# First heads of a hashed attention kernel: loads and row copies moved between queues and engines, clearings moved back, idle products on TensorE

## The chip, the cores and the metric
The kernel runs on one core of a Trainium2 chip. The metric is the device time of one execution in microseconds (us), the median of several runs. TensorE (PE) does the products, VectorE (DVE), ScalarE (ACT) and GpSimd (POOL) the elementwise work, and SyncE (SP) issues nearly all DMAs.

## The reference
```
q_bits, k_bits = (q @ proj > 0), (k @ proj > 0)        # 6 bits, a bucket number for each row
scores = where(q_bucket == k_bucket, q @ k.T / 8, -1e9)
attn = exp(scores - rowmax);  attn /= sum(attn) + 1e-9
x = attn @ v                                           # 2 batches x 8 heads, 768 rows, 64 columns
x = elu(x @ w_in) @ w_out                              # 1536 tokens, 512 -> 2048 -> 512
x = x + routed expert (top 1 of 8, 512 -> 1024 -> 512), for tokens with x @ w_skip > 0
```
All data are f32. Products that need more than one pass's precision are made of a rounded high part and a low part (the rest), both of type fp32r.

## The kernel before, in words
The 16 heads are worked one after the other, in a software pipeline in which the score products of head h stand beside the maxima of head h+1 and the transposes of head h+2. Each engine has an instruction list written out by hand; semaphores order them.

For one head the steps are these. SP loads q and k side by side into `qk_nat` (line 317, `load_qk`). PE transposes them into PSUM, six 128x128 transposes (unit T, line 1160). ACT rounds the transposed pair into `hi` (`round_qk`, line 656), and DVE subtracts it from the PSUM values into `lo` (`low_qk`, line 825). PE multiplies by the projection split into `pw[0]` and `pw[1]` (unit BITS, lines 1167 to 1169, six products of 384 columns), and DVE turns the signs into rows of +-numbers in `qb` and `kb` (`bits`, line 837, two instructions). Meanwhile six row copies move halves of `hi` and `lo` to other partitions, as DMAs on SP's queue: `copy_rows` (line 337) makes `qb`, `kb`, `qa`, `ka` from `hi`, and `copy_low_rows` (line 343) fills the other half of `qa` and `ka` from `lo`. PE then forms six tiles of hashed scores (units MAX, line 1176, two products each) from which DVE takes row maxima (`maximum`, line 845). DVE pads them (`row_maxima`, line 852), PE transposes them (MAX_T, line 1181) and DVE writes them negated into rows of `qb` (`minus_maxima`, line 858). Only then come the true score products (lines 1191, 1192), ACT's exponentials (line 673), and the products with v (lines 1207 to 1209).

All units T, BITS, MAX, MAX_T and SCORES share three pairs of PSUM banks in the order of `PSUM_ORDER`: a unit waits until the third unit before it has been consumed. Round `round_qk(h)` and `low_qk(h)` overwrite `hi` and `lo`, so both wait until all six row copies of head h-1 have landed (`rows_copied`, 16 for each DMA) and until BITS of h-1 is done.

Ahead of the steady pipeline stands a start: FIRST_UNITS on PE (T of head 0, BITS of head 0, T of head 1, six MAX of head 0, MAX_T, BITS of head 1), with DVE in the order `low_qk(0)`, `bits(0)`, `low_qk(1)`, six maxima. Before that, POOL makes the identity and constants (lines 461 to 480, `const_ready`), clears parts of `qb`, `kb` of heads 1 and 2 (line 486) and sets rows of ones (line 490), then clears or sets parts of `p_lo`, `v_hi`, `v_lo` (lines 493 to 497). DVE clears `pw` and the parts of head 0 (lines 800 to 804), and splits the projection into high and low parts, four times a pair of small instructions (lines 811 and 813). SP issues the loads in the order q0, k0, proj twice, q1, k1, v0, v1.

The functions in the program:

Of the kernel before, what the change touches and what calls it, by code (L numbers as in the profile page):

```python
# [5 lines left out]
F32 = mybir.dt.float32  # L6
# [5 lines left out]
ALU = mybir.AluOpType  # L12
ACT = mybir.ActivationFunctionType
AX = mybir.AxisListType

P = 128
# [3 lines left out]
QT = S // P  # L20
HALF = S // 2
BITS = 6
# [37 lines left out]
def head_units(h, s):  # L60
# [8 lines left out]

FIRST_UNITS = [("T", 0, 0), ("BITS", 0, 0), ("T", 1, 0)] + [("MAX", 0, t) for t in range(QT)] + \  # L70
              [("MAX_T", 0, 0), ("BITS", 1, 0)]


PSUM_ORDER = list(FIRST_UNITS)
# [6 lines left out]
def build(nc, q, k, v, proj, w_in, w_out, w_skip, w_gate, w1, w2, out, y_rows):  # L81
    ctx = ExitStack()
    with ctx:
# [132 lines left out]

        names = []

        names += "const_loaded gates_loaded const_step const_ready rows_ready proj_step proj_ready table_in consts2 row_step".split()

        names += "tq_done hi_done lo_done pj_done bits_done m_done max_done mx_ready mt_done neg_done".split()

        names += "v_high v_ready st_done exp_done p_hi_ready p_lo_dve p_lo_pool pv_done eps_ready od_ready".split()

# [29 lines left out]
        def pool_settled(eng):  # L254


            if eng is nc.gpsimd:
                eng.sem_inc(s_["pool_passed"], 1)

        def psum(kind, h, i):  # L260

# [50 lines left out]
        def _(sp):  # L312
            def load_qk(h):
                if h >= 2:
                    sp.wait_ge(s_["tq_done"], h - 1)
                for i, x in enumerate((q_h, k_h)):
                    sp.dma_start(qk_nat[h % 2][:, :, i, :], x[h]).then_inc(qk_loaded[h % 2], 16)

            def load_v(h):
# [10 lines left out]
            def copy_rows(h):  # L330
                i = h % 3
                if h >= 3:
                    sp.wait_ge(s_["st_done"], QT * (h - 2))
                sp.wait_ge(s_["hi_done"], h + 1)
                for dst, src in ((qb[i][0:D, :], hi[0:D, :]), (kb[i][0:D, :], hi[D:P, :]),
                                 (qa[i][D:P, :], hi[0:D, :]), (ka[i][0:D, :], hi[D:P, :])):
                    sp.dma_start(dst.bitcast(F32), src.bitcast(F32)).then_inc(rows_copied[i], 16)

            def copy_low_rows(h):
                i = h % 3  # L340
                sp.wait_ge(s_["lo_done"], h + 1)
                for dst, src in ((qa[i][0:D, :], lo[0:D, :]), (ka[i][D:P, :], lo[D:P, :])):
                    sp.dma_start(dst.bitcast(F32), src.bitcast(F32)).then_inc(rows_copied[i], 16)

            def load_den(pair):
# [18 lines left out]
                    .then_inc(s_["rden_loaded"], 16)  # L364

            load_qk(0)
            for half in range(2):
                sp.dma_start(pj[half * D:half * D + D, :], proj).then_inc(s_["const_loaded"], 16)
            load_qk(1)
            load_v(0)  # L370
            load_v(1)
# [88 lines left out]
        def _(pool):  # L460
# [20 lines left out]
                               fill=TINY, base=BITS - 1, pattern=[[0, 1]], channel_multiplier=-1)\  # L481
                .then_inc(s_["const_ready"], 1)
            pool.wait_ge(s_["const_ready"], 1)
            for i in (1, 2):
                for x in (qb[i], kb[i]):
                    done = pool.memset(x[D:P, :].bitcast(F32), 0.0)
                done.then_inc(s_["const_step"], 1)
                pool.wait_ge(s_["const_step"], 4 + i)
            for i in (1, 2):
                done = pool.memset(kb[i][NEG_ROW:NEG_ROW + QT, :].bitcast(F32), 1.0)  # L490
            done.then_inc(s_["rows_ready"], 1)
            pool.wait_ge(s_["rows_ready"], 2)
            pool.memset(p_lo[:, :, :, HALF:WIDE].bitcast(F32), 0.0)
            for u in range(2):
                at = D * (1 - u)
                pool.memset(v_hi[u][:, :, at:at + D].bitcast(F32), 1.0)
                done = pool.memset(v_lo[u][:, :, at:at + D].bitcast(F32), 0.0)
            done.then_inc(s_["const_step"], 1)
            pool.wait_ge(s_["const_step"], 7)

            def low_of_v(h):

# [146 lines left out]
        def _(act):  # L649
            def round_qk(h):  # L650

                act.wait_ge(s_["tq_done"], h + 1)
                if h:
                    act.wait_ge(rows_copied[(h - 1) % 3], 96 * ((h - 1) // 3 + 1))
                    act.wait_ge(s_["pj_done"], h)
                act.activation(hi[:, :].rearrange("p (b n) -> p b n", b=2), psum("T", h, 0), ACT.Copy)\
                    .then_inc(s_["hi_done"], 1)
# [26 lines left out]
            def outputs(h):  # L684
# [5 lines left out]
                if h >= 4:  # L690
                    act.wait_ge(s_["xt_ready"], (h - 4) // 2 + 1)
                act.activation(o_den[h % 4][:, :].rearrange("p (b n) -> p b n", b=2), ps_o, ACT.Identity,  # L692
                               bias=eps_sum[:, h % 2:h % 2 + 1]).then_inc(s_["od_ready"], 1)

            act.wait_ge(s_["const_ready"], 1)
            act.activation(table[:, :], thr[:, :], ACT.Copy).then_inc(s_["table_in"], 1)
            round_qk(0)
            round_qk(1)
            act.wait_ge(s_["const_step"], 7)
            high_of_v(0)  # L700
            high_of_v(1)

# [94 lines left out]
        def _(dve):  # L797
# [4 lines left out]
                dve.memset(x[D:P, :].bitcast(F32), 0.0).then_inc(s_["proj_step"], 1)  # L802
            dve.wait_ge(s_["proj_step"], 4)
            dve.memset(kb[0][NEG_ROW:NEG_ROW + QT, :].bitcast(F32), 1.0).then_inc(s_["rows_ready"], 1)
            dve.wait_ge(s_["const_loaded"], 32)

            for i, signs in enumerate(((1.0, -1.0), (-1.0, 1.0))):
                rows = slice(i * D, i * D + D)
                for n, sign in enumerate(signs):
                    at = slice(i * K_BITS + n * BITS, i * K_BITS + n * BITS + BITS)  # L810
                    dve.tensor_scalar(pw[0][rows, at], pj[rows, :], sign, None, ALU.mult).then_inc(s_["proj_step"], 1)
                    dve.wait_ge(s_["proj_step"], 4 + 2 * i + n + 1)
                    done = dve.scalar_tensor_tensor(pw[1][rows, at], pj[rows, :], sign, pw[0][rows, at].bitcast(F32),
                                                    ALU.mult, ALU.subtract)
            done.then_inc(s_["proj_ready"], 1)
# [3 lines left out]
            def low_qk(h):  # L819

                dve.wait_ge(s_["hi_done"], h + 1)
                if h:
                    dve.wait_ge(rows_copied[(h - 1) % 3], 96 * ((h - 1) // 3 + 1))
                    dve.wait_ge(s_["pj_done"], h)
                dve.tensor_tensor(lo[:, :].rearrange("p (b n) -> p b n", b=2), psum("T", h, 0),
                                  hi[:, :].rearrange("p (b n) -> p b n", b=2).bitcast(F32), ALU.subtract)\
                    .then_inc(s_["lo_done"], 1)

            def bits(h):

                i = h % 3
                dve.wait_ge(s_["pj_done"], h + 1)
                if h >= 3:
                    dve.wait_ge(s_["st_done"], QT * (h - 2))
                for dst, row in ((qb[i], 0), (kb[i], K_BITS)):
                    rows = slice(row, row + 2 * BITS)
                    done = dve.tensor_scalar(dst[BIT_ROW:BIT_ROW + 2 * BITS, :].rearrange("p (b n) -> p b n", b=2),  # L837
                                             psum("BITS", h, 0)[rows], thr[rows, 0:1], thr[rows, 1:2],
                                             ALU.is_ge, ALU.mult)
                done.then_inc(s_["bits_done"], 1)  # L840
# [37 lines left out]

            low_qk(0)
            bits(0)  # L880
            low_qk(1)
            for t in range(QT):
                maximum(0, t)
            row_maxima(0)
            minus_maxima(0)
            bits(1)
# [259 lines left out]
        def _(pe):  # L1146
# [7 lines left out]
            def prepare(kind, h, i):  # L1154
# [8 lines left out]
                elif kind == "BITS":  # L1163
                    pe.wait_ge(s_["lo_done"], h + 1)
                    for b in range(2):
                        half = slice(b * HALF, b * HALF + HALF)
                        pe.matmul(to[:, b, :], pw[0][:, :], hi[:, half], start=True, stop=False)
                        pe.matmul(to[:, b, :], pw[0][:, :], lo[:, half], start=False, stop=False)
                        mm = pe.matmul(to[:, b, :], pw[1][:, :], hi[:, half], start=False, stop=True)
                    mm.then_inc(s_["pj_done"], 1)  # L1170
                elif kind == "MAX":
                    if i == 0:
                        pe.wait_ge(s_["bits_done"], h + 1)
                        pe.wait_ge(rows_copied[h % 3], 96 * (h // 3 + 1))
                    for b in range(2):
                        mm = pe.matmul(to[:, b, :], qb[h % 3][0:NEG_ROW, i * P:i * P + P],  # L1176
                                       kb[h % 3][0:NEG_ROW, b * HALF:b * HALF + HALF], start=True, stop=True)
                    mm.then_inc(s_["m_done"], 1)
                else:
                    pe.wait_ge(s_["mx_ready"], h + 1)  # L1180
                    pe.transpose(to[:, 0, 0:P], mxp[:, :], ident[:, :]).then_inc(s_["mt_done"], 1)

            def scores(h, s):
# [2 lines left out]
                to = take("SCORES", h, s)  # L1186
                if s == 0:
                    pe.wait_ge(s_["neg_done"], h + 1)
                for b in range(2):
                    half = slice(b * HALF, b * HALF + HALF)  # L1190
                    pe.matmul(to[:, b, :], ka[i][:, s * P:s * P + P], qa[i][:, half], start=True, stop=False)  # L1191
# [20 lines left out]

            pe.wait_ge(s_["const_ready"], 1)
            for unit in FIRST_UNITS:
                if unit[0] == "BITS":
                    pe.wait_ge(s_["proj_ready"], 1)
                elif unit == ("MAX", 0, 0):
                    pe.wait_ge(s_["rows_ready"], 2)
                prepare(*unit)

            for n in range(QT * HEADS):
# [211 lines left out]
```

## Time and profile before

| | us |
|---|---|
| median of three runs | 685.39 |
| lowest and highest | 683.17, 687.35 |
| the profiled execution's own time | 682.89 |
| its span, first to last instruction | 681.1 |

The profile's page gives the busy time of each engine over the span, and then the span in 40 slices of 17 us each. It says that PE is busy for 643.4 us (94%), DVE for 53%, ACT for 48% and POOL for 37%. The first slice is the one that differs: PE is at 3 tenths there. The granted clock of TensorE is written in tenths of full speed. The chain of waits follows the work that ended last back to the start, and names for each stretch the engine and line that the end depended on. One line of a view can stand for several instructions (xN).

### The profile page before, as it was taken

Reading aid. Unit: us, or ns where it says so; the run is one execution under the profiler, and the core shown is the slowest. Engines: PE = TensorE matmul, PEld = TensorE weight load, DVE = VectorE, ACT = ScalarE, POOL = GpSimd, SP = SyncE. Lnnn points to the kernel's source line nnn. Section 1 sums busy time; section 2 is a strip of 40 time slices with the busy share of each in tenths; the row PEclk is TensorE's granted clock in tenths of the full one; section 3 lists DMA queues with packets and bytes.
Section 4 is the critical chain, followed back from the end, with each engine's and each line's share of the span. In section 5 each row is a group of like instructions: output and inputs, shape, how many; then the busy total and the mean of one; then the engine's idle time right before and its main releaser. Section 6 shows DMA issues by size and latency. Waiting matters only on the chain.

```text
span 681.1 us, 9823 instructions
## 1 busy us (share of the span) xinstructions
PE 643.4 (94%) x3632; PEld 595.0 (87%) x3632; DVE 360.5 (53%) x495; ACT 326.3 (48%) x505; POOL 249.1 (37%) x206
## 2 busy tenths in 40 slices
PE   3899999998989999999999999999999967999996
PEld 3699999898989999999999999999999857899995
DVE  6788777878788862565322222222322256455451
ACT  2277777676767776555423334333333320343330
POOL 5145587777686789340300030000013008221111
PEclk9699999999999999999999999999999976999999
DMA  7663474655465304511020002000367672999100
GB/s 171 147 146 87 123 171 123 164 144 149 120 165 125 90 20 147 152 61 60 1 93 0 1 0 92 0 0 0 154 246 247 246 278 66 358 360 337 50 12 25
DMA packets 67960, 84.00 MB, mean 123 GB/s; under 512 B 34260, under 2 KB 44500, under 8 KB 67920
## 3 DMA queue, kind: packets, MB, share of 16 engines
q1 hardware_dynamic: 66640, 79.83, 39.2%
q0 software_dynamic: 1280, 3.65, 1.7%
q8 instruction: 24, 0.39, 0.2%
q14 instruction: 16, 0.13, 0.1%
HBM read 56.64 MB, written 8.44 MB: 96 GB/s over the span
## 4 chain that ended last, share of the span: by engine, by line
PE 86%; DVE 7%; DMA 3%; issue 2%; ACT 1%; SPq 0%; POOL 0%; POOLq 0%; DVEq 0%; ACTq 0%
PE banks L1243 20%; PE banks L1254 19%; PE banks L1367 9%; PE banks L1382 6%; PE banks L1176 5%; PE banks L1207 4%; PE banks L1191 4%; PE banks L1209 4%; PE banks L1208 4%; PE banks L1192 4%; DVE row_max L845 2%; DMA y_rows<-y 2%; PE banks L1160 1%; DVE probs_lo L868 1%; PE banks L1272 1%
## 5 line engine op out<-in xcount | busy, mean ns | idle before, releaser
L1243 PE MATMUL banks<-x_hi,w_split 128*128 (+1 forms) x512 | 141.7, 337 | 0.0
L937 DVE SCALAR_TENSOR_TENSOR g<-exp_min_h,banks 128x384 f32<-128x384 f32 x64 | 35.4, 554 | 188.6 <-ACT exp_min_h L743 188.6
L514 POOL TENSOR_TENSOR probs_lo<-probs,probs_hi 128x768 fp32r<-128x768 f32 x64 | 109.8, 1731 | 57.3 <-ACT probs_hi L681 56.8
L1254 PE MATMUL banks<-w_split,g_hi 128*128 128x512 f32 x384 | 120.3, 394 | 0.1
L740 ACT ACTIVATE exp_min_h<-banks 128x384 f32<-128x384 f32 x64 | 31.5, 492 | 168.0 <-PE banks L1243 168.0
L673 ACT ACTIVATE probs<-banks 128x768 f32<-128x768 f32 x96 | 77.7, 809 | 60.8 <-PE banks L1192 60.7
L845 DVE TENSOR_REDUCE row_max<-banks 128x1 f32<-128x768 f32 x96 | 88.9, 950 | 29.3 <-PE banks L1176 29.2
L1243 PEld LDWEIGHTS banks<-x_hi,w_split 128*128 128x128 f32 x512 | 93.6, 188 | 2.7
L1243 PE MATMUL banks<-x_lo,w_split 128*128 (+1 forms) x256 | 86.0, 336 | 0.0
L1254 PEld LDWEIGHTS banks<-w_split,g_hi 128*128 128x128 f32 x384 | 70.6, 188 | 12.3 <-DVE g_lo L911 0.5
L681 ACT ACTIVATE probs_hi<-probs 128x768 fp32r<-128x768 f32 x96 | 80.6, 841 | 0.0
L1254 PE MATMUL banks<-w_split,g_lo 128*128 128x512 f32 x192 | 75.9, 396 | 0.0
L1191 PE MATMUL banks<-q_lo_hi_T,k_hi_lo_T 128*128 128x384 f32 x192 | 67.2, 350 | 2.8 <-DVE q_hi_rows_T L858 2.7
L1207 PE MATMUL banks<-probs_hi,v_hi_ones 128*128 128x386 f32 x192 | 66.4, 346 | 0.9 <-ACT o_and_den L692 0.9
L1192 PE MATMUL banks<-q_hi_rows_T,k_hi_rows_T 128*128 128x384 f32 x192 | 65.5, 341 | 0.0
L1208 PE MATMUL banks<-probs_lo,v_hi_ones 128*128 128x386 f32 x192 | 65.0, 339 | 0.0
L1209 PE MATMUL banks<-probs_hi,v_lo_zeros 128*128 128x386 f32 x192 | 64.9, 338 | 0.0
L1367 PEld LDWEIGHTS banks<-x_T,expert_w 128*128 128x128 f32 x512 | 60.9, 199 | 1.9 <-issue 1.3
L1367 PE MATMUL banks<-x_T,expert_w 128*128 128x128 f32 x512 | 61.1, 282 | 0.9 <-DVE x_T L1055 0.9
L1176 PE MATMUL banks<-k_hi_rows_T,q_hi_rows_T 96*128 96x384 f32 x192 | 52.7, 359 | 5.8 <-DVE k_hi_rows_T L837 3.8
L1243 PEld LDWEIGHTS banks<-x_lo,w_split 128*128 128x128 f32 x256 | 48.1, 188 | 2.7
L629 POOL DMA_INDIRECT out<-expert_out,scatter_rows x8 | 16.8, 2096 | 78.9 <-DVE expert_out L1111 78.9
(163 smaller groups left out, 1043.1 us busy)
## 6 DMA issues: line engine op xcount, KB each, us to landing
expert_w<-in_moe_w SPq DMA_DIRECT2D x32, 1024.0 KB, 7.0
w_raw<-in_moe_w_in SPq DMA_DIRECT2D x16, 256.0 KB, 4.1
w_raw<-in_moe_w_out SPq DMA_DIRECT2D x16, 256.0 KB, 5.3
qk_nat<-in_q SPq DMA_DIRECT2D x16, 192.0 KB, 3.9
qk_nat<-in_k SPq DMA_DIRECT2D x16, 192.0 KB, 5.8
v_nat<-in_v SPq DMA_DIRECT2D x16, 192.0 KB, 3.5
q_hi_rows_T<-qk_hi_T SPq DMA_DIRECT2D x16, 192.0 KB, 2.8
k_hi_rows_T<-qk_hi_T SPq DMA_DIRECT2D x16, 192.0 KB, 3.1
```

Source lines behind the costliest of these rows:

```text
L514: pool.tensor_tensor(p_lo[:, n % RING, :, 0:HALF], probs[:, n % RING, :].rearrange("p (b n) -> p b n", b=2), p_hi[:, n % RING, :, 0:HALF]. ...
L681: act.activation(p_hi[:, n % RING, :, 0:HALF], probs[:, n % RING, :].rearrange("p (b n) -> p b n", b=2), ACT.Copy).then_inc(s_["p_hi_ready ...
L845: dve.tensor_reduce(mx[:, t:t + 1], psum("MAX", h, t), AX.XY, ALU.max).then_inc(s_["max_done"], 1)
L1176: mm = pe.matmul(to[:, b, :], qb[h % 3][0:NEG_ROW, i * P:i * P + P], kb[h % 3][0:NEG_ROW, b * HALF:b * HALF + HALF], start=True, stop=True)
L1191: pe.matmul(to[:, b, :], ka[i][:, s * P:s * P + P], qa[i][:, half], start=True, stop=False)
L1192: mm = pe.matmul(to[:, b, :], kb[i][:, s * P:s * P + P], qb[i][:, half], start=False, stop=True)
L1207: pe.matmul(to, v_hi[h % 2][:, t, :], high, start=(t == 0), stop=False)
L1208: pe.matmul(to, v_hi[h % 2][:, t, :], low, start=False, stop=False)
L1209: mm = pe.matmul(to, v_lo[h % 2][:, t, :], high, start=False, stop=(t == QT - 1))
L1243: mm = pe.matmul(banks[:, j % 2, 0:BN], w, x, start=(c == 0 and w is hi and x is x_hi), stop=(c == KC - 1 and w is lo))
L1254: mm = pe.matmul(banks[:, 2 + t, :], g, W[:, j, part, :], start=(j == 0 and i == 0), stop=(j == FT - 1 and i == 2))
L1367: mm = pe.matmul(banks[:, j // 4, j % 4 * P:j % 4 * P + P], w1_sb[:, r, c, j * P:j * P + P], xeT[:, e % 2, c, :], start=(c == 0), stop=(c ...
```

## The change
The change touches only the start of the kernel, up to the first heads.

* The loads of k for heads 0 and 1 are issued on ACT's queue, not SP's. The projection is loaded by one DMA that writes both halves.
* ACT, not DVE, makes the four high parts of the projection; DVE keeps the four low parts.
* Of the six row copies of head 0, POOL makes the one for `qb` and ACT the one for `kb` by instructions (`first_rows`), SP issues two as DMAs and ACT's queue issues two (`ka`). The two that the maxima need are thus no DMAs. For head 0 `rows_copied` is expected to reach 64 (and 32 less than 96 a round in all later uses of that semaphore), through the new helper `copied`.
* POOL clears and sets `p_lo`, `v_hi` and `v_lo` first, then makes its row copy, and only then clears `qb`, `kb` of heads 1 and 2.
* DVE does `low_qk(1)` after the first maximum of head 0, not before it.
* PE makes idle products, 128x128 by 128x128 in f32 of the identity with itself, into PSUM bank 7, whose values nobody reads: 8 before T of head 0, 8 before BITS of head 0, 8 before the first MAX, 2 before each of the five others, and 4 before MAX_T. They wait for nothing but `const_ready`.

```diff
+IDLE_WORK = {("T", 0, 0): 8, ("BITS", 0, 0): 8, ("MAX", 0, 0): 8}
+IDLE_WORK.update({("MAX", 0, t): 2 for t in range(1, QT)})
+IDLE_WORK["MAX_T", 0, 0] = 4
+        def copied(h):
+            return rows_copied[h % 3], 96 * (h // 3 + 1) - (32 if h % 3 == 0 else 0)
 # SP
-                for i, x in enumerate((q_h, k_h)):
+                for i, x in enumerate((q_h, k_h) if h >= 2 else (q_h,)):
+                    if h == 0 and n != 2:
+                        continue
-                for dst, src in ((qa[i][0:D, :], lo[0:D, :]), (ka[i][D:P, :], lo[D:P, :])):
+                for dst, src in ((qa[i][0:D, :], lo[0:D, :]), (ka[i][D:P, :], lo[D:P, :]))[:1 if h == 0 else 2]:
-            for half in range(2):
-                sp.dma_start(pj[half * D:half * D + D, :], proj).then_inc(s_["const_loaded"], 16)
+            with nc.allow_non_contiguous_dma(reason="small"):
+                sp.dma_start(pj[:, :], proj.unsqueeze(0).broadcast_to([2, D, BITS])).then_inc(s_["const_loaded"], 16)
 # GpSimd: p_lo, v_hi, v_lo first, then
+            pool.wait_ge(s_["const_step"], 5)
+            pool.wait_ge(s_["rows_ready"], 1)
+            pool.wait_ge(s_["hi_done"], 1)
+            pool.tensor_scalar(qb[0][0:D, :], hi[0:D, :].bitcast(F32), 1.0, 1.0, ALU.mult, ALU.mult)                .then_inc(s_["first_rows"], 1)
             for i in (1, 2):
                 for x in (qb[i], kb[i]):
                     done = pool.memset(x[D:P, :].bitcast(F32), 0.0)
...
 # ACT
+            for h in range(2):
+                act.dma_start(qk_nat[h][:, :, 1, :], k_h[h]).then_inc(qk_loaded[h], 16)
             act.wait_ge(s_["const_ready"], 1)
             act.activation(table[:, :], thr[:, :], ACT.Copy).then_inc(s_["table_in"], 1)
+            act.wait_ge(s_["const_loaded"], 16)
+            act.wait_ge(s_["proj_step"], 4)
...
+                    act.activation(pw[0][rows, at], pj[rows, :], ACT.Copy, scale=sign).then_inc(s_["proj_high"], 1)
             round_qk(0)
+            act.wait_ge(s_["rows_ready"], 1)
+            act.wait_ge(s_["hi_done"], 1)
+            act.activation(kb[0][0:D, :], hi[D:P, :].bitcast(F32), ACT.Copy).then_inc(s_["first_rows"], 1)
+            act.dma_start(ka[0][0:D, :].bitcast(F32), hi[D:P, :].bitcast(F32)).then_inc(rows_copied[0], 16)
+            act.wait_ge(s_["lo_done"], 1)
+            act.dma_start(ka[0][D:P, :].bitcast(F32), lo[D:P, :].bitcast(F32)).then_inc(rows_copied[0], 16)
             round_qk(1)
 # DVE
-                    dve.tensor_scalar(pw[0][rows, at], pj[rows, :], sign, None, ALU.mult).then_inc(s_["proj_step"], 1)
-                    dve.wait_ge(s_["proj_step"], 4 + 2 * i + n + 1)
+                    dve.wait_ge(s_["proj_high"], 2 * i + n + 1)
-            low_qk(1)
             for t in range(QT):
                 maximum(0, t)
+                if t == 0:
+                    low_qk(1)
 # PE
             for unit in FIRST_UNITS:
+                for _ in range(IDLE_WORK.get(unit, 0)):
+                    pe.matmul(banks[:, 7, 0:P], ident[:, :], ident[:, :], start=True, stop=True)
...
                 elif unit == ("MAX", 0, 0):
-                    pe.wait_ge(s_["rows_ready"], 2)
+                    pe.wait_ge(s_["rows_ready"], 1)
```

## Rows read from the trace of the kernel before
**Rows 1.** The page: busy times, PE's slices, the granted clock, the chain by engine.
```profile
PE 643.4 (94%) x3632; PEld 595.0 (87%) x3632; DVE 360.5 (53%) x495; ACT 326.3 (48%) x505; POOL 249.1 (37%) x206
PE   3899999998989999999999999999999967999996
PE 86%; DVE 7%; DMA 3%; issue 2%; ACT 1%; SPq 0%; POOL 0%; POOLq 0%; DVEq 0%; ACTq 0%
```
**Rows 2.** Windows: start:end, length, busy us of each engine (instructions), PEclk, DMA, GB/s.
```profile
5.00:10.00 5.00, 1.38 (x7) 1.01 (x6) 4.44 (x9) 0.81 (x1) 3.50 (x8) 1.00 0.88 235
20.00:25.00 5.00, 3.37 (x11) 3.19 (x11) 3.34 (x5) 0.00 (x0) 0.00 (x0) 0.50 0.86 170
35.00:40.00 5.00, 4.99 (x29) 4.86 (x29) 4.88 (x7) 3.29 (x5) 1.76 (x2) 1.00 0.71 143
```
**Rows 3.** The chain of waits in order of time: start us, us, what.
```profile
7.25 1.40 DVE proj_both_hi L811
...
10.37 3.85 DMA k_hi_lo_T<-qk_lo_T
...
16.10 5.19 DVE row_max L845 x6
...
27.29 1.28 PE banks L1160 x6
...
41.50 0.66 PE banks L1160 x6
...
49.95 0.26 PE banks L1167
...
51.08 0.11 PE banks L1181
```
**Rows 4.** Timeline of the start: start us, us, engine, line, instruction, idle before.
```profile
2.40 0.18 POOL L480 TENSOR_SCALAR_AFFINE_SELECT bit_thresholds<-bit_thresholds 32x1 f32<-32x1 f32 x1
2.61 0.20 ACT L696 ACTIVATE table_in<-bit_thresholds 128x2 f32<-128x2 f32 x1 [0.56 <-POOL bit_thresholds L480]
...
4.84 1.51 PE L1160 MATMUL banks<-ident,qk_nat 128*128 128x128 f32 x6 [4.84 <-DMA qk_nat<-in_k]
6.39 0.81 ACT L656 ACTIVATE qk_hi_T<-banks 128x768 fp32r<-128x768 f32 x1 [3.58 <-PE banks L1160]
...
9.97 0.66 PE L1167 MATMUL banks<-qk_hi_T,proj_both_hi 128*128 128x384 f32 x1 [3.62 <-DVE qk_lo_T L825]
12.27 1.07 DVE L837 TENSOR_SCALAR q_hi_rows_T<-banks,bit_thresholds 12x768 fp32r<-12x768 f32 x1 [2.44 <-PE banks L1169]
14.68 0.93 PE L1176 MATMUL banks<-k_hi_rows_T,q_hi_rows_T 96*128 96x384 f32 x4 [1.17 <-DVE k_hi_rows_T L837]
...
24.05 1.07 DVE L837 TENSOR_SCALAR q_hi_rows_T<-banks,bit_thresholds 12x768 fp32r<-12x768 f32 x1 [0.99 <-PE banks L1169]
26.31 0.98 PE L1176 MATMUL banks<-k_hi_rows_T,q_hi_rows_T 96*128 96x384 f32 x2 [1.01 <-issue]
28.60 0.81 ACT L656 ACTIVATE qk_hi_T<-banks 128x768 fp32r<-128x768 f32 x1 [2.46 <-PE banks L1160]
29.45 0.96 DVE L825 TENSOR_TENSOR qk_lo_T<-banks,qk_hi_T 128x768 fp32r<-128x768 f32 x1 [1.17 <-ACT qk_hi_T L656]
```
**Rows 5.** Windows again, of line 1367 alone (f32 products of 128 columns): PE, PEld, PEclk, DMA.
```profile
567.80:573.20 5.40, 5.37 (x25) 5.40 (x26) 0.50 0.02 5
573.40:577.00 3.60, 3.60 (x35) 3.60 (x33) 1.00 0.42 131
```
**Rows 6.** Windows: before the clock's fall, at its rise, and among pauses (columns as Rows 2).
```profile
13.51:16.95 3.44, 1.54 (x6) 0.94 (x6) 2.72 (x4) 1.63 (x3) 1.28 (x2) 1.00 0.78 144
30.50:31.00 0.50, 0.50 (x3) 0.50 (x4) 0.48 (x1) 0.50 (x2) 0.00 (x0) 0.89 0.83 190
190.98:194.39 3.41, 2.01 (x11) 1.40 (x9) 3.33 (x4) 2.16 (x4) 3.35 (x3) 1.00 0.63 141
```
**Rows 7.** The page's groups: line, engine, instruction xcount | busy us, mean ns.
```profile
L547 POOL TENSOR_SCALAR x_hi<-attn_T 128x768 fp32r<-128x768 f32 x8 | 7.8, 975 | 88.7 <-PE banks L1243 88.5 <-POOLq L538 0.2
```

## What the change is expected to do
> **What bounds the kernel now.** I read the page first: PE is busy for 94% of the span and carries 86% of the chain, and its only thin slice of the first 31 is the first, at 3 tenths [rows 1]. From 35 us on PE has no pause [rows 2], so what the start takes is handed on: if the steady pipeline begins d us earlier, the end should come d us earlier. The windows show what is wrong with the start: from 20 to 25 us PE is busy for 3.37 us of 5 and at a granted clock of 0.50 (the 1.2 GHz level); at 35 us it is at 1.00 [rows 2].
>
> The chain of waits names the links. They are: the small DVE instructions that split the projection, of which the last high part takes 1.40 us; the last row copy, 3.85 us from issue to landing, after which `hi` and `lo` of head 1 may be written; six maxima in 5.19 us, 0.865 each; and then products and transposes at half clock [rows 3]. The timeline gives the times at which each step starts [rows 4]; I take the new schedule from those.
>
> **Durations at either clock.** Six transposes take 1.28 us in the chain at 27.29 and 0.66 at 41.50 [rows 3]. BITS cold lasts from 9.97 until DVE starts on it at 12.27, 2.30 us [rows 4]; at full clock its six products take from 49.95 to 51.08, 1.13 us [rows 3], and with some 0.2 for the hand-over 1.33. An idle product is f32 with 128 columns, of the kind of line 1367, which leaves two records a product: 5.40 / 25 = 0.216 a record cold, 3.60 / 35 = 0.103 warm [rows 5]. So a product costs 0.43 or 0.21, and eight of them 3.46 or 1.65.
>
> **The clock.** It rose in the window at 30.5, after PE had worked without a pause since 26.31 [rows 4, 6], 4.2 us. The four MAX products from 14.68 take 0.93 together [rows 4], 0.23 each against 0.32 cold, so it had also risen just before, behind the products that began at 9.97. It had fallen by 20 [rows 2], behind a stretch in which PE was busy for 1.54 us of 3.44 [rows 6]. With the change PE starts at `const_ready`, 2.58 [rows 4], and has no pause until BITS. I take it that the clock has risen before BITS starts (9.5 below).
>
> **The change, part by part.**
>
> *Projection and k loads.* The last low part waited for a high part that ended at 7.25 + 1.40 = 8.65 [rows 3]. ACT's four small copies lie between 0.20 each, its own smallest instruction, and 1.40, DVE's dearest [rows 3, 4]. I take 0.20, the same engine's; they are then done before T is, and next late is `lo` of head 0. At 1.40 they would end near 10.5 and BITS would be 1 us later. The k loads on ACT's queue could bring T forward: it started when k had landed, at 4.84 [rows 4]. Between nothing and the 0.7 us of one issue; but the idle products cover either, so zero.
>
> *Eight idle products before T.* 2.65 + 3.46 = 6.1, 1.3 us after T could start before. T itself cold: 1.28 + 0.25 for the hand-over, so ACT's `hi` starts at 7.65 (before 6.39 [rows 4]), ends 8.46, and DVE's `lo` runs 8.5 to 9.46 at 0.96. This part costs; it is paid back by the clock.
>
> *Eight before BITS.* From 7.4 PE fills the gap until `lo`: warm 1.65, done at 9.05; if up to 0.9 us of it is still cold it is done by 9.5. BITS starts at 9.55 (before 9.97) and takes 1.33 instead of 2.30: DVE's `bits(0)` starts at 10.9 (12.27), ends at 13.0. Gain so far 1.4.
>
> *Eight before MAX.* T of head 1 ends at 11.5 (10.9 less 0.2, plus 0.66), the idle products at 13.15. MAX waits for `bits(0)` at 13.0 plus 0.26: equal. Were they cold, MAX would be late by 1.8 us.
>
> *The two row copies for the maxima.* ACT's is 64x768 behind `hi`, 0.81 by the same engine's `hi` [rows 4], done at 9.3. POOL's: its tensor_scalar of 128x768 takes 0.98 [rows 7]; between 0.5 and 2 us, done by 10.5 at worst. MAX needs both at 13.0: hidden, even at 2 us. POOL's six late clearings, at 0.98 each (the dearer instruction), end at 16.4, ahead of `bits(1)` at 21.8: hidden.
>
> *The other four, and `low_qk(1)` behind a maximum.* Issued on two queues at 8.5, 9.3, 9.5 and 9.9. The last took 3.85 before, in a full queue [rows 3]; at that it lands at 13.8. ACT's `hi` of head 1 then ends at 14.6. Maximum 0 of head 0 runs 13.85 to 14.75, so `lo` of head 1 (0.96) follows without a gap to 15.7, and five maxima end at 15.7 + 5 x 0.865 = 20.05. Before they ended at 16.10 + 5.19 = 21.29 [rows 3]. Gain 1.25. What ends last here is DVE, and PE's idle pairs (0.41 + 0.35 a tile) fit in its 0.865.
>
> *MAX_T, BITS 1, `bits(1)`.* Before, `bits(1)` started at 24.05, 2.76 behind the last maximum [rows 3, 4]. Warm, BITS saves 0.97 of that: start 21.8. Gain 2.25. The four idle products before MAX_T are done while DVE still works.
>
> *MAX and T in head 0's loop.* Before, from MAX at 26.31 to `hi` of head 2 at 28.60, 2.29 us [rows 4]. Warm: 0.35 + 0.66 + 0.2 = 1.2. Gain 3.35 at `lo` of head 2, which stood at 29.45 [rows 4] and now stands at 26.1. From there DVE's five maxima bound both kernels and PE is saturated behind them. I take the whole as **3.2 us**, leaving 0.15 for waits I have not seen. On the profiled execution: 682.89 - 3.2 = 679.7. The median of the runs lies 2.5 above that execution, so in medians 685.39 - 3.2 = **682.2**.
>
> **Rivals.**
>
> *The copies of head 0 land late (20%).* Copies that SP alone issued stood ahead of q2 and k2 in one queue; now `ka`'s last copy is in ACT's queue, beside q2 and k2 in SP's. Four copies of 0.197 MB and two loads of the same size are 1.18 MB; at 235 GB/s [rows 2] that is 5.0 us from 9.2, with the latency 14.8. Then `hi` of head 1 ends at 15.6, `lo` at 16.6, and 0.9 us are lost: gain 2.3, 683.1. For it: the DMA engines are at 0.88 in this stretch [rows 2]. Against: before, six copies were in flight and the last still took only 3.85. The Trainium skill, "DMA: Bandwidth & Descriptors", section "Issuing engines are not separate DMA queues", says that transfers run on the same 16 engines and interleave whatever engine started them, and that a second issuer only saves issue time. By that rule it is 683.1 and not 682.2; no run here shows two queues at once.
>
> *The clock falls again behind the maxima (22%).* From about 22.5 to 24.0 PE has nothing (there are no idle products there): it waits for `bits(1)`. Around this gap, from 22.2 to 25.6, it works for some 1.8 us (the end of SCORES, 0.3; MAX and T, 1.0; SCORES again, 0.5). It fell behind 1.54 of 3.44 us and stayed through 2.01 of 3.41 [rows 6]; this lies between. Then MAX and T of the loop are cold and the last 1.1 us aren't gained: 2.1, 683.3; if it falls already before BITS 1, another 1.0, 684.3. What follows is cold in both kernels until PE again has no pause.
>
> *The clock comes too late; slower (6%).* If PE's idle products don't bring it up before MAX, they are a burden. T at 6.1, eight cold ones end at 10.9, BITS 2.30 to 13.2, `bits(0)` ends 15.3; T of head 1 ends at 14.1, eight more at 17.6, MAX starts at 17.6 against 14.68. Each further tile costs PE 2 x 0.43 + 2 x 0.32 = 1.5 us against DVE's 0.865, the sixth ends at 25.6, four idle ones at 27.3, where MAX_T was at 21.6: 5.7 us slower, 691.1. It decides from the point at which BITS starts: each us of lateness there passes on. Against it: twice before, products without a pause did raise the clock.
>
> *The start is earlier, but the end isn't (8%).* Something behind sets the pace, such as the loads of w: 685.4. Against: PE has no pause from 35 us on [rows 2].
>
> **Numbers.** Full gain 44%, 682.2, its own range 680.5 to 684. With the rivals 20, 22, 6 and 8%. Two changes are apart when they differ by over 0.5%, 3.4 us, which is about what a measurement of this kernel can tell. The forecast lies just inside that bound (below 681.96 is faster), so the spread of the measurement, three runs over 4.2 us before, splits the first case in two. Faster 0.42, same 0.52, slower 0.06. The range, 679.8 to 685.8, takes in the rivals but the slower one.
>
> **What would show it.** In the changed kernel: T at about 6.1; a granted clock of 1.00 (or BITS products 0.18 apart) from 9.5 on; `bits(0)` at 10.9; the first maximum at 13.85; the sixth ending at 20.05; `bits(1)` at 21.8; `lo` of head 2 at 26.1. If ACT's second `hi` starts after 14, the copies are late. If the six transposes behind 24 us take 1.3 us, the clock has fallen. Wrong would be BITS products 0.32 apart, a MAX that starts later than 14.7, or all steps early and a span of 681 still.

## The result, and the profile after

| | before | changed |
|---|---|---|
| median, us | 684.28 (683.06 to 687.35, 4 runs) | 676.90 (676.18 to 677.66, 4 runs) |
| ratio | | 0.9886 [0.9846, 0.9925] |
| span of the profiled execution | 681.1 | 674.3 |

The gain is 7.4 us where I had forecast 3.2, and the time lies below my range. The mechanism of the start came out nearly as written. What I missed is not at the start: between 60 and 265 us there are waits whose number and length change from one execution to the next, and the first comparison caught the two kernels with different amounts of them. Medians here and below are over all runs; three single runs that lie over 1.5% above the fastest of their kernel (693.08, 689.87 and 686.7) are left out of the ratios.

The page of the changed kernel, the same lines as [rows 1]: PE's first slice has gone from 3 tenths to 7, and little else has moved.

```profile
PE 645.4 (96%) x3708; PEld 599.5 (89%) x3708; DVE 355.0 (53%) x491; ACT 327.6 (49%) x510; POOL 249.6 (37%) x207
PE   7899999999998999999999999999999968999995
PE 87%; DVE 5%; DMA 3%; issue 2%; ACT 1%; POOL 0%; POOLq 0%; SPq 0%; DVEq 0%; ACTq 0%
```

Windows of the changed kernel (columns as [rows 2]). From 20 to 25 us the granted clock is 1.00 where it was 0.50, and it stays there through the gap before `bits(1)` is done, with PE busy for 3.62 us of 5. In the stretch that the rival named, 22.2 to 25.6 us, PE worked for 2.02 us of 3.40 (1.8 forecast) at 1.00. So the clock did not fall behind the maxima.

```profile
5.00:10.00 5.00, 4.70 (x35) 4.54 (x35) 1.44 (x5) 2.26 (x6) 1.95 (x3) 1.00 0.68 161
20.00:25.00 5.00, 3.62 (x21) 3.03 (x22) 3.76 (x4) 0.82 (x2) 0.00 (x0) 1.00 0.71 150
```

Its chain of waits through the start (start us, us, what; the links of [rows 3]). The idle products open it and T follows at once, in 0.67 us, so the clock had risen by 6.3. The last row copy is in it still, 4.55 us from issue to landing; six maxima have become five behind it; T and BITS at 37.81 and 46.26 answer to those at 41.50 and 49.95 in the kernel before.

```profile
2.64 3.64 PE banks L1258 x16
6.29 0.67 PE banks L1197 x6
...
7.92 0.97 DVE qk_lo_T L859
8.91 4.55 DMA k_hi_lo_T<-qk_lo_T
...
15.33 4.33 DVE row_max L881 x5
...
24.30 0.67 PE banks L1197 x6
...
37.81 0.65 PE banks L1197 x6
...
46.26 0.26 PE banks L1204
```

Its timeline, the steps of [rows 4] (start us, us, engine, line, instruction, idle before).

```profile
6.98 0.81 ACT L674 ACTIVATE qk_hi_T<-banks 128x768 fp32r<-128x768 f32 x1 [0.97 <-PE banks L1197]
...
7.88 0.84 ACT L729 ACTIVATE k_hi_rows_T<-qk_hi_T 64x768 fp32r<-64x768 f32 x1
...
8.00 0.83 POOL L506 TENSOR_SCALAR q_hi_rows_T<-qk_hi_T 64x768 fp32r<-64x768 f32 x1 [3.81 <-ACT qk_hi_T L674]
...
9.03 0.41 PE L1204 MATMUL banks<-qk_hi_T,proj_both_hi 128*128 128x384 f32 x1 [0.30 <-DVE qk_lo_T L859]
...
10.35 1.07 DVE L873 TENSOR_SCALAR q_hi_rows_T<-banks,bit_thresholds 12x768 fp32r<-12x768 f32 x1 [1.47 <-PE banks L1206]
...
12.76 0.58 PE L1216 MATMUL banks<-k_hi_rows_T,q_hi_rows_T 96*128 96x384 f32 x2
...
13.38 0.96 DVE L881 TENSOR_REDUCE row_max<-banks 128x1 f32<-128x768 f32 x1 [0.88 <-PE banks L1216]
...
13.53 0.81 ACT L674 ACTIVATE qk_hi_T<-banks 128x768 fp32r<-128x768 f32 x1 [4.81 <-DMA k_hi_lo_T<-qk_lo_T]
...
21.45 1.07 DVE L873 TENSOR_SCALAR q_hi_rows_T<-banks,bit_thresholds 12x768 fp32r<-12x768 f32 x1 [0.16 <-PE banks L1206]
...
25.83 0.96 DVE L859 TENSOR_TENSOR qk_lo_T<-banks,qk_hi_T 128x768 fp32r<-128x768 f32 x1 [0.54 <-ACT qk_hi_T L674]
```

`lo` of head 2 starts at 25.83 against 29.45: 3.62 us. T is at 37.81 against 41.50, BITS at 46.26 against 49.95: 3.69 both times. That is all that the start gives. But the first `g` (line 937 before, 974 changed), which opens the stage behind the attention, starts at 262.06 against 268.72, 6.66 us earlier. So 3.0 us come from the heads in between, whose code the change does not touch.

```profile
262.06 0.56 DVE L974 SCALAR_TENSOR_TENSOR g<-exp_min_h,banks 128x384 f32<-128x384 f32 x1 [6.74 <-ACT exp_min_h L778]
268.72 0.55 DVE L937 SCALAR_TENSOR_TENSOR g<-exp_min_h,banks 128x384 f32<-128x384 f32 x1 [6.75 <-ACT exp_min_h L743]
```

**Where the other 3 us are.** I looked for PE's idle time between 60 us and the end of the attention. Before there are 7.8 us in 11 pauses of over 0.15 us, in the changed kernel 4.9 in 6. One in the kernel before, read back. GpSimd normalises a pair of heads (line 535) and waits 1.68 us for `rden_rows`, the inverse sums broadcast from DRAM. It starts at 122.25. DVE's two low parts of the probabilities (line 868) start at 124.16 beside it and take 3.50 us; `minus_maxima` (line 858) comes behind them, and PE waits for it.

```profile
122.25 4.59 POOL L535 TENSOR_TENSOR attn_T<-o_and_den,rden_rows 64x768 f32<-64x768 f32 x2 [1.68 <-DMA rden_rows<-den_rows]
124.16 3.50 DVE L868 TENSOR_TENSOR probs_lo<-probs,probs_hi 128x768 fp32r<-128x768 f32 x2
127.69 0.95 DVE L858 TENSOR_TENSOR q_hi_rows_T<-banks,minus_diag 6x768 fp32r<-6x768 f32 x1
...
128.79 0.41 PE L1191 MATMUL banks<-q_lo_hi_T,k_hi_lo_T 128*128 128x384 f32 x1 [0.43 <-DVE q_hi_rows_T L858]
```

The same place in the changed kernel: the wait is 0.27, the normalisation ends at 120.36, the low parts start at 120.30 and take 1.81.

```profile
116.54 3.82 POOL L551 TENSOR_TENSOR attn_T<-o_and_den,rden_rows 64x768 f32<-64x768 f32 x2 [0.27 <-DMA rden_rows<-den_rows]
120.30 1.81 DVE L904 TENSOR_TENSOR probs_lo<-probs,probs_hi 128x768 fp32r<-128x768 f32 x2
122.14 0.95 DVE L894 TENSOR_TENSOR q_hi_rows_T<-banks,minus_diag 6x768 fp32r<-6x768 f32 x1
```

I call a pair of low parts of 3.3 us or more a slow pair. Both traces have a further one behind the last head, at 258.53 and 251.87, which every trace has and which is left out of the counts. Before has 3, the changed kernel 1. The Trainium skill, "SBUF — State Buffer", section "SBUF: two separate sides", says that VectorE and GpSimd share one pair of ports as an exclusive lock, which an operation of VectorE with two SBUF inputs wants when GpSimd reads SBUF, and that the loser is blocked for the whole instruction. By that rule the low parts are blocked behind a running normalisation; the trace agrees (3.50 against 1.81 us, and 4.59 against 3.82 for the two instructions of GpSimd).

The count of slow pairs does not show everything. First, a slow pair need not overlap the normalisation. The one at 156.49 starts as the normalisation ends and runs beside GpSimd's own low part:

```profile
156.49 3.32 DVE L868 TENSOR_TENSOR probs_lo<-probs,probs_hi 128x768 fp32r<-128x768 f32 x2
157.28 1.71 POOL L514 TENSOR_TENSOR probs_lo<-probs,probs_hi 128x768 fp32r<-128x768 f32 x1 [0.75 <-ACT probs_hi L681]
```

Second, a wait for the broadcast load can cost time without any slow pair. In the changed kernel the normalisation waits 1.05 us and ends at 150.90. VectorE's padding of the maxima (line 888), which also has two SBUF inputs and takes 0.17 at 19.69, runs beside it for 1.36 us. The pair behind it is fast, but late:

```profile
147.06 3.84 POOL L551 TENSOR_TENSOR attn_T<-o_and_den,rden_rows 64x768 f32<-64x768 f32 x2 [1.05 <-DMA rden_rows<-den_rows]
149.55 1.36 DVE L888 SCALAR_TENSOR_TENSOR row_max_pad<-row_max 128x6 f32<-128x6 f32 x1
150.84 1.81 DVE L904 TENSOR_TENSOR probs_lo<-probs,probs_hi 128x768 fp32r<-128x768 f32 x2
```

### The profile page after: what moved, and what is told of

Read it like the earlier page. It is cut to its first block, busy times and chain, and to the rows that moved or that the text cites. A ratio compares the mean times of both kernels' runs of the same rounds, so it can differ in the third digit from the quotient of the medians.

```text
span 674.3 us, 9979 instructions
## 1 busy us (share of the span) xinstructions
PE 645.4 (96%) x3708; PEld 599.5 (89%) x3708; DVE 355.0 (53%) x491; ACT 327.6 (49%) x510; POOL 249.6 (37%) x207
## 4 chain that ended last, share of the span: by engine, by line
PE 87%; DVE 5%; DMA 3%; issue 2%; ACT 1%; POOL 0%; POOLq 0%; SPq 0%; DVEq 0%; ACTq 0%
PE banks L1287 20%; PE banks L1298 20%; PE banks L1411 9%; PE banks L1426 7%; PE banks L1216 5%; PE banks L1249 4%; PE banks L1251 4%; PE banks L1250 4%; PE banks L1233 4%; PE banks L1234 4%; DMA y_rows<-y 2%; DVE row_max L881 1%; PE banks L1197 1%; PE banks L1316 1%; DVE probs_lo L904 1%
## 5 line engine op out<-in xcount | busy, mean ns | idle before, releaser
L1216 PE MATMUL banks<-k_hi_rows_T,q_hi_rows_T 96*128 96x384 f32 x192 | 51.3, 348 | 4.8 <-DVE k_hi_rows_T L873 2.9
```

## The experiments

Theory A: the start gives 3.2 to 3.7 us, part of it by the clock and part by the earlier copies; the rest of the difference is the number of slow pairs, which depends on when the broadcast load lands (from its issue to the end of GpSimd's wait) and varies by itself. Rival B: the clock brings both. Rival C: the moved DMAs leave the queues in another state, and by that later loads land sooner.

### Idle products alone

```diff
 # the kernel before, with IDLE_WORK as in the change
             for unit in FIRST_UNITS:
+                for _ in range(IDLE_WORK.get(unit, 0)):
+                    pe.matmul(banks[:, 7, 0:P], ident[:, :], ident[:, :], start=True, stop=True)
```

> The kernel before with the idle products alone. Theory A (the start gives 3.7 us, half of it by the clock; the rest of the gain is that the broadcast load of the inverse sums lands before VectorE's pair of low parts, so that GpSimd's normalisation no longer holds it up): BITS of head 0 starts near 9.9 as before, but the products are 0.18 us apart; the second round of hi still waits for the row copies until about 14.2, so the last maximum of head 0 ends near 21.3; then the clock saves 0.9 and 1.1 us, and lo of head 2 starts near 27.4, 2.0 us earlier. The later stalls are those of the kernel before, since nothing behind the start differs: 682.3 against 684.3. Theory B (the later gain is brought by the clock too): 679 or less. Theory C (the row copies and the queue bring the later gain): like A here.

Measured: 683.37 (680.18 to 688.01) against 685.19 for the kernel before (25 runs, 678.78 to 688.01 and one of 693.08), ratio 0.9986 [0.9953, 1.0019], which is not clearly faster. `lo` of head 2 starts at 29.26, only 0.2 us earlier and not the 2.0 of my expectation. Its chain shows why (start us, us, what): T waits behind the idle products, the row copies are issued that much later, and the last lands at 15.62. The first MAX waits for it and is cold again, 0.98 for two products.

```profile
6.42 1.29 PE banks L1164 x6
...
11.72 3.91 DMA k_hi_lo_T<-qk_lo_T
...
15.76 0.98 PE banks L1180 x2
...
27.14 0.59 PE banks L1180 x2
```

### All but the idle products

```diff
 # the changed kernel
-                for _ in range(IDLE_WORK.get(unit, 0)):
-                    pe.matmul(banks[:, 7, 0:P], ident[:, :], ident[:, :], start=True, stop=True)
```

> The changed kernel without its idle products. Theory A: T of head 0 starts as soon as k has landed (4.8), BITS cold from about 8.3, maxima end near 19.7, but everything up to lo of head 2 is cold: lo of head 2 near 27.8, 1.7 us earlier than before and 2 us later than with the idle products. The later stalls are few, as in the changed kernel, if they hang on what the other parts changed: 679. Theory B (the clock brings the later gain): 682.5. If more stalls come back, the number of pairs of low parts over 3 us says so.

Measured: 683.77 (678.72 to 687.04), ratio 0.9981 [0.995, 1.0012], again not clearly faster. `lo` of head 2 starts at 28.22, 1.2 us earlier. Against the expectation the trace has four slow pairs, not few: what the moves changed does not keep them away. The chain: T starts when k has landed, and everything to the first MAX is cold.

```profile
0.77 4.24 DMA qk_nat<-in_k
...
5.14 1.53 PE banks L1197 x6
...
13.45 0.99 PE banks L1216 x2
```

### One queue

```diff
 # the changed kernel
-            for h in range(2):
-                act.dma_start(qk_nat[h][:, :, 1, :], k_h[h]).then_inc(qk_loaded[h], 16)
...
-            act.dma_start(ka[0][0:D, :].bitcast(F32), hi[D:P, :].bitcast(F32)).then_inc(rows_copied[0], 16)
-            act.wait_ge(s_["lo_done"], 1)
-            act.dma_start(ka[0][D:P, :].bitcast(F32), lo[D:P, :].bitcast(F32)).then_inc(rows_copied[0], 16)
 # and all four on SP's queue, as before
```

> The changed kernel with all DMAs on SP's queue again (k loads of heads 0 and 1 and the two ka copies of head 0). Theory A: T starts at 6.1 as before behind the idle products, the copies land within 0.5 us of the changed kernel's 13.5, hidden behind the first maximum; within 0.5 us of 676.9 in the start. Theory C (the use of ACT's queue leaves SP's rings in another state, and by that the later loads land sooner): the later stalls come back, 680.

Measured: 679.17 (675.48 to 686.7), ratio 0.9924 [0.9882, 0.9965]. `lo` of head 2 at 26.49, 0.66 later than in the changed kernel's first trace and within 0.2 of its second (26.68), so ACT's queue is worth nothing in the start; one slow pair. The later stalls did not come back in the trace, which speaks against rival C. The median is no help: it lies near C's 680, but the changed kernel with ACT's queue, taken again below, has 678.90. The runs now spread over 8 us and more, where the first four of the changed kernel spread over 1.5, and the trace is of one of the faster.

### The early store

SP issues the store of the inverse sums before the two low row copies, and so the broadcast load earlier.

```diff
                     copy_rows(h + 2)
-                    copy_low_rows(h + 2)
                 if h % 2 and h >= 3:
                     store_rden(h // 2 - 1)
+                if h + 2 < HEADS:
+                    copy_low_rows(h + 2)
+                if h % 2 and h >= 3:
                     load_rden(h // 2 - 1)
```

> The kernel before, with the store of the inverse sums issued ahead of the two low row copies and not behind them, so that the broadcast load is issued some 1.5 us earlier. Theory A: it lands before GpSimd waits for it or up to 1.5 us sooner; the three pairs of low parts of 3.3 to 3.5 us in the kernel before come down to 1.8 in two or three cases, and 2 to 4 us are gained with the start unchanged: 681. Rival (the wait for the load isn't what makes the later stalls, or another load comes late in its place): 684.3, no change.

Measured: 676.93, and 676.36 to 677.11 in all runs, ratio 0.9891 [0.9844, 0.9938]. One order of issues in the kernel before is worth more than I had expected, and the four runs lie within 0.8 us, where 24 of the 25 of the plain kernel lie within 9.2 (678.78 to 688.01). At the place shown above GpSimd no longer waits, and the pair is fast (one wait is left in the trace, 0.47 us at 179.91). PE's pauses between 60 and 265 us are down from 7.8 us to 2.5 in 3.

```profile
120.28 3.84 POOL L537 TENSOR_TENSOR attn_T<-o_and_den,rden_rows 64x768 f32<-64x768 f32 x2
124.06 1.81 DVE L870 TENSOR_TENSOR probs_lo<-probs,probs_hi 128x768 fp32r<-128x768 f32 x2
```

This gives a clean ground on which the change can be measured. The next four have it or stand beside it.

### The change with the early store, and again without

> The changed kernel with the early store of the inverse sums. The kernel before with it took 676.93 with no slow pair of low parts but the last. Theory A (the start gives 3.7, the slow pairs are a lottery that both kernels draw from, and the early store takes it away): first g at 229.1 where the kernel before with the early store has it at 232.8 in ... its own trace less 3.6, and 673.3. Rival (the changed kernel had already avoided the slow pairs by itself, so the two gains overlap): 675.5 to 676.5.

> The changed kernel once more, unaltered, beside the others. Theory A: its slow pairs vary from execution to execution as those of the kernel before do (678.8 to 693 there), so its median now lies between 677 and 681.5, near 685.2 - 3.7 = 681.5 at the high end. Rival (the change itself lowers the number of slow pairs): 676 to 678 in all executions.

Measured: with the early store 673.53 (672.27 to 674.1), where theory A said 673.3 and the rival 675.5 or more. The changed kernel as it is: 678.90 (674.66 to 682.16), beside 681.81 (678.45 to 683.87, 16 runs) for the kernel before, ratio 0.9961 [0.9937, 0.9986]. The 7.4 us of the first comparison are 2.9 here (2.7 by the ratio). The rival, 676 to 678 in all runs, is out: the ten runs spread over 7.5 us.

### The two halves on the clean ground

> The kernel before with the idle products and the early store: the idle products by themselves, without the lottery. By the trace of the idle products alone, where lo of head 2 starts at 29.26 against 29.45: 676.93 - 0.2 = 676.7. Rival (the clock alone brings its 2 us): 675.

> The changed kernel without idle products, with the early store. By its trace, lo of head 2 at 28.22 against 29.45: 676.93 - 1.2 = 675.7. With the changed kernel's 673.3 the idle products are then worth 2.4 us on top of the moves, against 0.2 without them. Rival (each part is worth the same with and without the other): 675.1 or less.

Measured: idle products alone 675.52 (674.43 to 676.54), moves alone 675.45 (674.15 to 678.0). The first misses its expectation of 676.7 and lies between it and the rival's 675; the second was expected at 675.7. The traces tell the halves better than these medians of few runs; below, by `lo` of head 2.

### Again on one chip, and a dose

Four more kernels were run on one chip: before and changed with the early store; the kernel before with the broadcast load issued later; and the changed kernel with the early store and 4 idle products ahead of T, not 8.

```diff
 # late load, in the kernel before
                     load_qk(h + 3)
+                if h % 2 == 0 and h >= 4:
+                    load_rden(h // 2 - 2)
...
                     store_rden(h // 2 - 1)
-                    load_rden(h // 2 - 1)
+                    if h == HEADS - 1:
+                        load_rden(h // 2 - 1)
 # fewer idle products first, in the changed kernel with the early store
-IDLE_WORK = {("T", 0, 0): 8, ("BITS", 0, 0): 8, ("MAX", 0, 0): 8}
+IDLE_WORK = {("T", 0, 0): 4, ("BITS", 0, 0): 8, ("MAX", 0, 0): 8}
```

> The kernel before with the early store, once more, on one chip with the next one. Theory A: 676.9 again, whatever the plain kernel before takes on this chip (684.3, 685.2 and 681.8 so far).

> The changed kernel with the early store, once more. Theory A: 3.4 us under the one before it (673.5), the gain of the change without the lottery, and close to the 3.2 of the prediction. Rival (the 7.4 us of the first comparison were all due to the change): 669.5.

> The kernel before with the broadcast load of the inverse sums issued behind the next head's loads of q and k, so that it is later by their issue and their transfer, 1.3 us or more. Theory A: GpSimd's wait for it grows in every pair, five pairs of low parts take over 3.3 us, and the kernel is slower than before by 3 us or more with the same start. Rival (the wait is without effect on the end): no change, 682 to 685.

> The changed kernel with the early store and 4 idle products ahead of the first T, not 8. T then starts when k has landed, at 4.8 and not 6.1; the clock comes up behind T, before BITS, as PE still has no long pause; the row copies and both rounds of hi and lo are up to 1.3 us earlier: 672.4 against 673.5. Rival (the clock comes later because PE waits between the idle products and T): BITS at half clock, 674 or more.

Measured, beside 683.35 (22 runs) for the kernel before: 675.86 (11 runs), 672.79 (6 runs), 685.82 with the ratio 1.0043 [1.0007, 1.0079], and 671.68 with the ratio 0.9846 [0.9804, 0.9888]. The change on the clean ground is worth 675.86 - 672.79 = 3.1 us (expected 3.4); by the spread of the 11 and the 6 runs I estimate some 1.3 us either way. The late load costs 2.5 us by the medians and 2.9 by the ratio, a little less than the 3 or more expected. It brought all five pairs to 3.3 us and over; one of them, with a wait of 2.35:

```profile
93.01 4.51 POOL L538 TENSOR_TENSOR attn_T<-o_and_den,rden_rows 64x768 f32<-64x768 f32 x2 [2.35 <-DMA rden_rows<-den_rows]
94.84 3.49 DVE L871 TENSOR_TENSOR probs_lo<-probs,probs_hi 128x768 fp32r<-128x768 f32 x2
```

The 11 runs of the kernel before with the early store spread from 674.48 to 679.12 on this chip, so it does not look as if the early store removed the late landing altogether; in the seven traces with it three waits are left, of 0.34, 0.47 and 0.97 us, all near 180 us. And the fewer idle products: T starts at 5.21 when k has landed, cold, and the clock is up all the same before BITS, whose products start at 8.84 and then 0.16 to 0.25 us apart (0.32 cold). The 1 us is kept to the end: 0.9 to 1.0 by the first `g`, 1.1 by the medians. It is the best version that was run.

```profile
5.21 1.55 PE banks L1199 x6
...
8.72 4.64 DMA k_hi_lo_T<-qk_lo_T
...
15.23 4.33 DVE row_max L883 x5
...
24.19 0.67 PE banks L1199 x6
```

All traces side by side. `lo` 2 is the start of the low part of head 2, the end of the start; `g` the first `g`; the difference holds heads 1 to 15.

| kernel | `lo` 2 | `g` | difference | slow pairs |
|---|---|---|---|---|
| before | 29.45 | 268.72 | 239.3 | 3 |
| changed | 25.83 | 262.06 | 236.2 | 1 |
| changed again | 26.68 | 263.10 | 236.4 | 1 |
| one queue | 26.49 | 262.21 | 235.7 | 1 |
| no idle products | 28.22 | 269.76 | 241.5 | 4 |
| idle products alone | 29.26 | 272.99 | 243.7 | 5 |
| late load | 29.74 | 275.61 | 245.9 | 5 |
| before, early store (twice) | 29.64, 29.57 | 262.43, 262.30 | 232.8, 232.7 | 0 |
| idle products alone, early store | 28.86 | 261.19 | 232.3 | 0 |
| no idle products, early store | 27.99 | 261.23 | 233.2 | 0 |
| changed, early store (twice) | 26.56, 26.78 | 258.97, 259.10 | 232.4, 232.3 | 0 |
| the same, 4 idle products first | 25.73 | 258.06 | 232.3 | 0 |

With no slow pair the heads take 232.3 to 233.2 whatever the start was. The 233.2 belongs to the one early-store trace with a wait of 0.97 us, which puts 15.68 us between the low parts at 166.81 and 182.49, where the same step is 14.86 in the changed kernel with the early store: 0.8 us lost without a slow pair. The rest of the table, against 232.4, is 2.3 to 4.0 us a slow pair, and the high quotients are those of the traces with only one. In the first trace of the changed kernel the waits of 1.05 and 0.91 us without a slow pair cost 0.9 and 0.8 (steps of 15.75 and 15.63 against 14.84 and 14.86), and the slow pair at 211.31, with its wait of 2.51, costs 2.1 (31.48 us from the low parts before it to those behind it, against 29.42). So what counts is how late the load lands; the slow pair is its dearest form.

What the halves are worth on the clean ground is therefore read from `lo` 2, ahead of all such waits: idle products alone 0.7 to 0.8 us, moves alone 1.6, both 2.8 to 3.1. Together they are worth 0.5 to 0.7 us more than their sum. (By the first `g` it would be 1.1 to 1.2 each and 3.2 to 3.5 for both, but the waits of 0.97, 0.47 and 0.34 us are in that.) The trace of the idle products alone shows one side of this: T is later, and the DMA copies hand that on to the maxima; with the copies for the maxima made by ACT and GpSimd, they no longer do.

## Why the prediction was wrong, point by point

**The start was right in mechanism and size.** Forecast 3.35 by its own steps, cut to 3.2; measured 3.6 to 3.7 in the first trace, and on the clean ground 2.8 to 3.1 at `lo` of head 2 and 3.2 to 3.5 at the first `g` (262.43 less 258.97, 262.30 less 259.10). In the first trace BITS started at 9.03 (9.55 forecast), `bits(0)` at 10.35 (10.9), the first maximum at 13.38 (13.85), the last maximum ended at 19.66 (20.05), `bits(1)` started at 21.45 (21.8), `lo` of head 2 at 25.83 (26.1). Nearly the whole offset at BITS is one term: "T itself cold: 1.28". The clock had risen by 6.3 there, after 3.6 us of products, and T took 0.67. When the clock rises varies: in the three later traces of the same start T took 1.29, 1.26 and 1.29, and `lo` began at 8.68, 8.65 and 8.67, where I had put it at 8.5. Of the 3.6 us of the first trace some 0.7 to 0.9 were this luck, as `lo` of head 2 stood at 26.56 to 26.78 in the later three. The same start, in the changed kernel taken again (start us, us, what):

```profile
6.42 1.29 PE banks L1197 x6
7.74 0.82 ACT qk_hi_T L674
8.68 0.97 DVE qk_lo_T L859
9.67 4.63 DMA k_hi_lo_T<-qk_lo_T
...
14.38 0.82 ACT qk_hi_T L674
```

**POOL's copy, ACT's small copies and the clearings were hidden**, as written: 0.83 us for GpSimd's copy, 0.63 for all four of ACT's, the clearings done at 13.2.

**The copies of head 0 were late by half of what the rival said.** The last took 4.55 to 4.63 us and not the 3.85 that I used, and landed at 14.3 where T was cold (13.8 forecast, 14.8 by the rival); `lo` of head 1 then started at 15.2, not 14.75. That is 0.45 us, and it is the better part of why `lo` of head 2 stood at 26.6 to 26.8 there and not at 26.1. (The rival's 14.8 holds 0.6 us of latency for which it names no row.) The clock did not fall, nor come too late.

**The step that failed is the first one**: "From 35 us on PE has no pause [rows 2], so what the start takes is handed on", with the sum then set against a median as if all behind the start were fixed. The row on which it rests ends at 40 us, and says nothing of what follows. In the same trace PE has 7.8 us of pauses between 60 and 265, which the page's slices of 17 us show only as an 8 or a 9 [rows 1]. I used the sentence again against the rival "the start is earlier, but the end isn't". The spread of the three runs, 4.2 us, was taken as the error of a measurement; it is in the main how late the broadcast load lands. The kernel before spread over 9.2 us in 24 of 25 runs on one chip, and over 0.8 in the four with the early store there; on another over 9.5 in 21 of 22, and over 4.6 in eleven with the early store. My range was built from the start's unknowns alone and had nothing for this. What the runs show in place of the step: 3.0 of the 6.7 us by which the first `g` comes earlier arise behind the start, in those waits, and in the same two kernels compared again only 2.9 us are left in all.

**What the change is worth.** 3.1 us on the clean ground (0.5%), 2.9 in ten runs against sixteen, near the 3.2 forecast. The 7.4 of the first comparison were 3.6 of the start and the rest in waits for the broadcast load: as far as the later runs tell, a lucky draw of four runs.

**What stays open.** Whether the change by itself makes slow pairs rarer. The one-queue variant, whose start is nearly that of the changed kernel, was 5.2 us faster than the kernel before by the ratio on one chip [0.9882 to 0.9965], the changed kernel 2.7 on another [0.9937 to 0.9986]; the intervals meet. The three traces with this start and no early store have one slow pair each, the four with another start 3, 4, 5 and 5: few, but all one way. Nothing in the traces shows a cause for such an effect, as the broadcast load is issued 7.3 to 7.5 us ahead of the next `lo` in four of the five pairs of the kernel before and of the changed one. Nor do I know why its landing varies. Before: issued at 109.94, waited for until 122.25.

## What to carry to other kernels

Before a gain at the start is handed on to the end, look at the pauses of the bounding engine in every stage behind it, and ask which of them hang on a transfer that lands close to when it is wanted; a spread of a per cent between runs can be such a place, as here, and be worth more than the change under study. A small reorder of DMA issues that takes the place away first gives a ground on which small changes can be measured at all. Idle products that raise the clock cost what they delay: eight ahead of T cost 1 us against four, and alone, with the row copies still DMAs behind them, they gained 0.2 to 0.8 us.

## What the runs showed of the hardware that I had not expected

* The granted clock in the windows is 1.00 from the start, although six transposes at 4.84 take 1.51 us in the kernel before [rows 2, 4] and 0.82 in the changed one at 6.12. Ahead of the first change on record the column says nothing; the spacing of the products does.
* A pair of GpSimd multiplications that runs beside a pair of VectorE subtractions of two SBUF tiles stretches the latter from 1.81 to 3.50 us, and is itself stretched from 3.82 to 4.59. VectorE's small operation on `row_max` (128x6, both inputs in SBUF) goes from 0.17 to 1.36 us beside it.
* A broadcast load of 384 KB out of two rows of 3 KB in DRAM was waited for until 12 us after its issue, with q's and k's loads behind it.
